# Gated scan, token mixer and two MLPs in one kernel: state sums in groups of 32 columns, and a new order of VectorE's and ScalarE's work in the weave

## The reference, cut to what matters

```
x = attn(q, k, v, a_re, a_im)            # 4 batches, 8 heads, 768 steps, 48 channels a head
    # per step t: S = a[t] * S + k[t] v[t]^T ; y[t] = q[t] . Re(S)   (a complex, |a| capped at 0.999)
x = x as [batch, 768, 384]
u = x + (relu(x^T w_tok1) w_tok2)^T      # token mixer, 768 -> 256 -> 768
x2 = u + relu(u w_ch1) w_ch2             # channel MLP 1, 384 -> 1536 -> 384
xn = (x2 - mean) / sqrt(var + 1e-6) * g
out = x2 + relu(xn w2_ch1) w2_ch2        # channel MLP 2
```

## Time and profile before

| | |
|---|---|
| median of three executions | 917.45 us (915.28 to 918.37) |
| the profiled execution | 917.37 us |
| its span, first to last instruction | 915.6 us |
| TensorE busy | 846.4 us, 92% |
| VectorE busy | 475.3 us, 52% |
| ScalarE busy | 415.0 us, 45% |
| GpSimd busy | 26.1 us, 3% |
| mean granted TensorE clock | 0.983 |

### The profile page before, as it was taken

How to read it: one execution, slowest core, us unless ns; L and a number is a source line. 1 busy time by engine, 2 the same in 40 slices (tenths; PEclk the granted TensorE clock), 3 DMA queues, 4 the chain that set the end, 5 groups by cost and what they waited for, 6 DMA issues and landing times. The chain is left out here.

```text
span 915.6 us, 15179 instructions
## 1 busy us (share of the span) xinstructions
PE 846.4 (92%) x6280; PEld 822.7 (90%) x6280; DVE 475.3 (52%) x821; ACT 415.0 (45%) x767; POOL 26.1 (3%) x39
## 2 busy tenths in 40 slices
PE   0757888999999999999999999999999999999998
PEld 0546777999999999999999999999999999999997
DVE  5875568877757775676673454253223313322121
ACT  6766358777727767657663332232112211211111
POOL 1010000000000000000000000000000000000000
PEclk9977899999999999999999999999999999999999
DMA  9935964444524555516342610000001002000000
GB/s 369 178 64 89 240 167 77 81 78 118 101 68 78 103 96 142 105 25 128 65 88 36 232 53 1 1 1 1 26 26 53 27 1 78 1 27 27 1 26 26
DMA packets 46839, 71.07 MB, mean 78 GB/s; under 512 B 5040, under 2 KB 38064, under 8 KB 46256
## 3 DMA queue, kind: packets, MB, share of 16 engines
q1 hardware_dynamic: 46768, 70.09, 32.6%
HBM read 42.86 MB, written 8.26 MB: 56 GB/s over the span
## 5 line engine op out<-in xcount | busy, mean ns | idle before, releaser
L701 ACT ACTIVATE hidden<-bank 128x384 fp32r<-128x384 f32 x192 | 93.7, 488 | 325.1 <-PE bank L333 324.7
L1015 DVE SCALAR_TENSOR_TENSOR hidden<-bank,hidden 128x384 fp32r<-128x384 f32 x192 | 105.8, 551 | 258.3 <-ACT hidden L701 258.3
L331 PE MATMUL bank<-ch,hidden 128*128 128x384 f32 x576 | 192.7, 335 | 3.7 <-DVE x_u L1023 3.6
L333 PE MATMUL bank<-ch,hidden 128*128 128x384 f32 x576 | 192.8, 335 | 0.0
L332 PE MATMUL bank<-ch,hidden 128*128 128x384 f32 x576 | 192.4, 334 | 0.0
L331 PEld LDWEIGHTS bank<-ch,hidden 128*128 128x128 f32 x576 | 108.1, 188 | 4.9 <-issue 4.8
L332 PEld LDWEIGHTS bank<-ch,hidden 128*128 128x128 f32 x576 | 108.1, 188 | 0.0
L333 PEld LDWEIGHTS bank<-ch,hidden 128*128 128x128 f32 x576 | 108.1, 188 | 0.0
L331 PE MATMUL bank<-turned_x,ch 128*128 128x384 f32 x288 | 102.9, 357 | 1.7 <-DVE turned_x L1097 1.7
L332 PE MATMUL bank<-turned_x,ch 128*128 128x384 f32 x288 | 97.1, 337 | 0.0
L333 PE MATMUL bank<-turned_x,ch 128*128 128x384 f32 x288 | 97.0, 337 | 0.0
(11 more groups left out here) (168 smaller groups left out, 1468.6 us busy)
## 6 DMA issues: line engine op xcount, KB each, us to landing
rows<-hats SPq DMA_DIRECT2D x126, 128.5 KB, 4.7
a_t<-in_a_rows_dram SPq DMA_DIRECT2D x20, 384.0 KB, 5.5
qk_t<-in_qk_rows_dram SPq DMA_DIRECT2D x19, 384.0 KB, 5.7
v_t<-in_v_cols_dram SPq DMA_DIRECT2D x24, 192.0 KB, 5.5
plain_ch<-in_moe_w_ch_dram SPq DMA_DIRECT2D x6, 768.0 KB, 10.6
out_dram<-x_u SPq DMA_DIRECT2D x24, 192.0 KB, 2.0
x_kept_dram<-x_u SPq DMA_DIRECT2D x18, 192.0 KB, 3.8
x_u<-x_kept_dram SPq DMA_DIRECT2D x18, 192.0 KB, 3.1
```

Of the source, the lines that this page charges most:

```text
L331: nc.tensor.matmul(ps, lhs_h, rhs_h, start=first, stop=False, skip_group_check=True)
L333: return nc.tensor.matmul(ps, lhs_l, rhs_h, start=False, stop=final, skip_group_check=True)
L701: nc.scalar.activation(hid_h[:, m % NHID, :], hid_ps[m % 2][:, 0:HALF], ACT.Relu).then_inc(hidden_rounded, 1)
L1015: nc.vector.scalar_tensor_tensor(out=hid_l[:, m % NHID, :], in0=hid_ps[m % 2][:, 0:HALF], scalar=0.0, in1=hid_h[:, m % NHID, :].bitcast(F3 ...
```

## The change

Three edits, on three engines.

TensorE: `chunk_state` cuts the 96 columns of each head in three groups of 32, and each group writes its own 32 partitions of the bank. 160 products become 480.

VectorE, in the slots: `turn_scan(n+1)` goes ahead of `mask(n,0)` (but in slot 6); `turns_wrapped` keeps its place behind step 0; in slots j = 3 `add_u` goes from behind the second step's `rest_hidden` to a place between `turns_wrapped` and `mask(n,1)`; `row_stats` and the `rest_x` of the even tiles go behind `log_sums`, ahead of the fourth step.

ScalarE, in the slots: the `round_x` of slots j = 3 and j = 5 go behind `log_magnitude`, ahead of `keep_x`; in slot 6 `keep_khat(n,1)` goes ahead of the table load, `angle` and the sines.

```diff
+    GROUP = P // 4
@@ ScalarE, slot
                 step(0)
                 keep_khat(n, 0)
+                if n == NT:
+                    round_piece(act, 5)
+                    growth(n + 1 - PAIRS)
+                    keep_khat(n, 1)
+                    use_turns()
+                    angle(n + 1 - PAIRS)
+                    step(1)
+                    prepare(n + 1, round_turns, sines)
+                else:
+                    prepare(n + 1, round_turns)
+                    step(1)
+                    prepare(n + 1, sines)
+                    keep_khat(n, 1)
+                prepare(n + 1, decays)
+                step(2)
+                use_logs()
+                prepare(n + 2, square, inverse_of_re, log_magnitude)
                 if j == ST:
                     for i in range(0, ST, 2):
                         round_x(b * NT + i)
                 if j == NT - 1:
                     round_x(b * NT + j - 1)
-                if n == NT:
-                    round_piece(act, 5)
-                    growth(n + 1 - PAIRS)
-                    use_turns()
-                    angle(n + 1 - PAIRS)
-                    step(1)
-                    prepare(n + 1, round_turns)
-                else:
-                    prepare(n + 1, round_turns)
-                    step(1)
-                prepare(n + 1, sines)
-                keep_khat(n, 1)
-                prepare(n + 1, decays)
-                step(2)
-                use_logs()
-                prepare(n + 2, square, inverse_of_re, log_magnitude)
                 keep_x(n, slow)
@@ VectorE, slot
-                mask(n, 0)
                 if n == NT:
+                    mask(n, 0)
                     step(0)
                     rest_piece(dve, 5)
                     mask(n, 1)
                     prepare(n + 1, turn_scan, turns_wrapped)
                 else:
                     prepare(n + 1, turn_scan)
+                    mask(n, 0)
                     step(0)
+                    prepare(n + 1, turns_wrapped)
                     if j == ST:
-                        for i in range(0, ST, 2):
-                            rest_x(b * NT + i)
-                    if j == NT - 1:
-                        rest_x(b * NT + j - 1)
-                    prepare(n + 1, turns_wrapped)
+                        add_u(2 * (b - 1))
                     mask(n, 1)
                 step(1)
                 prepare(n + 1, grown_qk, turn_hats)
                 ...
                 prepare(n + 2, log_sums)
+                if j == ST:
+                    row_stats(2 * (b - 1))
+                    for i in range(0, ST, 2):
+                        rest_x(b * NT + i)
+                if j == NT - 1:
+                    rest_x(b * NT + j - 1)
                 step(3)
@@ VectorE, the steps of the weave
-                            if m - first == FT + 1:
-                                add_u(2 * b)
-                            if m - first == FT + 2:
-                                row_stats(2 * b)
@@ TensorE, chunk_state
-                    last = nc.tensor.matmul(m_ps[0:D2, h * D:(h + 1) * D], khat[:, h * D2:(h + 1) * D2], v_head(n, h), start=True, stop=True)
+                    for lo in range(0, D2, GROUP):
+                        last = nc.tensor.matmul(m_ps[lo:lo + GROUP, h * D:(h + 1) * D], khat[:, h * D2 + lo:h * D2 + lo + GROUP], v_head(n, h),
+                                                start=True, stop=True)
```

## The result

| | before | after |
|---|---|---|
| median, timed side by side | 917.08 us (4 runs) | 906.66 us (4 runs, 906.01 to 908.63) |
| ratio, 95% interval | | 0.9891 (0.9868 to 0.9914) |
| profiled execution | 917.37 us | 906.01 us |
| its span | 915.6 us | 904.2 us |
| mean granted TensorE clock | 0.983 | 0.980 |

The change is worth 1.1%, 10.4 us by the medians. In a second session, on another chip, the same kernel took 906.26 us (4 runs) against 915.08 (9 runs): 0.9901 (0.9885 to 0.9917), 8.8 us. In the changed kernel the lines have moved by one to six: `turn_k` is L1248, `scores` L1257, `outputs` L1275 and L1279, `chunk_state` L1290, `mask` L956, `rest_hidden` L1021, `add_u` L1029, `up` and `down` L332 to L334, `lay_rows` L472.

The account below looks back on a forecast made before the run. TensorE's own work was taken to bound the weave, with a hats-and-DMA loop nearly as long. Sums 3.85, `add_u` 5.4, `turn_scan` 1.1, less 0.4 and 0.6, make 9.35 us: 917.37 to 908.0, range 905.5 to 914.5.

Parts of the forecast that it names:

- The second loop: Tile start, second scores, mask, hats, then 7.7 to 8.8 us of DMAs: nearly as long as TensorE's own loop.
- State sums in groups of 32: TensorE's state sums: 45 ns a round of three groups, 0.72 us for 16 rounds, 0.50 us saved a tile.
- Plain slots: Slots 10, 14, 16, 22 save the full 0.50, 2.0 us; the other four only their slack, 1.2 us.
- `add_u`: Slots 9, 15, 21: ahead of the second mask it removes TensorE's wait; 1.8 us each, 5.4 together.
- `turn_scan`: Ahead of the first mask: hats about 0.55 us earlier in slots 12 and 18, 1.1 for both; plain slots 0.
- Slot 6: The wait for `keep_khat` goes, but the copy delays the angle, hats and start of tile 7: 0.4 us lost.
- Slots 11, 17, 23: `rest_x` ahead of the fourth `rest_hidden` exceeds its 0.4 us of cover: 0.2 us lost each, 0.6 together.
- The prologue: State sums before the weave: 0.5 us saved after tile 4, some 0.15 elsewhere.
- rival (1): State sums: pairs come no faster than 29 ns, 915.2 us, or 26 ns, 912.9 us; chance 0.20 for both.
- Rival (2): Late landings take half the gain of plain slots and `add_u`: 911 to 912 us; chance 0.12.
- Rival (3): State sums: the three groups run one after the other, each sum 0.9 us longer, 924.6 us; chance 0.08.
- Rival (4): State sums: weight loads alone set the step, 31 ns, 906.8 us; chance 0.05.

Follow-up runs that it names:

- the second version beyond the change: The changed kernel with `grown_qk` ahead of the second mask (but in slot 6), `keep_khat(6,1)` and the `rest_x` of slots 11, 17, 23 put back: 902.70 us, 0.9870.
- The first version beyond the change: The changed kernel with `grown_qk` moved ahead of the second mask in all slots but 6: 904.03 us, 0.9871 of before.
- the third: The second version beyond the change, with the second step's `rest_piece` in slots 6 and 7 moved behind the hats: 899.46 us, 0.9821 of before.

## Why the prediction was right, and where its terms were off

The forecast was 908.0 with a range of 905.5 to 914.5, the profiled execution took 906.01 and the median was 906.66. The likeliest case came out, by its own steps, and 2 us better. Those 2 us are luck: 1.9 us of the prologue's gain go with the clock (below). Without them the profiled executions differ by 9.5 us, against a sum of 9.35; and this sum is so close because a term that was 0.9 too small (`turn_scan`) met a loss of 0.7 in slot 7 that had been put at nothing.

**The second loop.** The prediction's main claim was that tile start, second mask, hats and landing form a loop nearly as long as TensorE's own. It holds: every start from tile 7 to tile 22, but for tiles 12 and 18, now comes 0.045 us after its landing, halving the DMAs' bytes brings the plain slots to 18.1, and so does an earlier hat. In the plain slots its waits are too short to be counted in the view of waits (0.6 us from 250 us on, at the starts of tiles 13 and 19): the reader finds them only as a distance, 18.13 to 18.40 where TensorE's own work is 18.1. The waits of `turn_k` between 160 and 500 us grew to 2.4, about 2.5 having been forecast, but not by the forecast's reason: 1.8 of them stand ahead of tile 8 (0.5 before), and the plain slots add none that the view counts.

**State sums in groups of 32.** Forecast 0.72 us from first to last start, 0.50 saved. Measured 0.675 and 0.57. A round of three groups takes 42 to 43 ns instead of 45. That is the size of the moving side as scaled from `scores`; no run varied the moving columns, so that it is what binds fits and is not shown. The rest is the two ends: 0.152 at the entry (0.15 forecast) and 0.136 at the exit (0.15). TensorE's own loop of 18.64 - 0.50 = 18.14 came out at 18.07.

**Plain slots.** Forecast 2.0 for slots 10, 14, 16 and 22, and 1.2 for 8, 13, 19 and 20. Measured 1.6 and 1.45 (of it 0.32 in slot 8). The sum is right and the split isn't. Slot 14 had a slack of 0.9 and saved only 0.26, since the DMAs of tile 15 landed 8.41 us after their hats instead of 7.87. Slot 20 had none and saved 0.38, since those of tile 21 took 8.36 instead of 8.76.

These shifts are not noise. Tile 15's landing comes 8.36 to 8.42 us after its hats in all seven executions with groups of 32, full DMAs and `grown_qk` where it was, and 7.87 and 7.80 in the two kernels with whole sums. The traces show something that goes with it: packets of 16 KB on the profile's queue for instructions, 49 of them before and 54 in the changed kernel, which has 640 matmuls more. The DMA view from the end of the hats on, for tile 15 before (316.40 to 322.40 us) and after (311.47 to 317.47):

```profile
q1 hardware_dynamic: 835, 0.78, 99.7%
```

```profile
q1 hardware_dynamic: 826, 0.77, 96.5%
q8 instruction: 1, 0.02, 1.8%
```

Of the 34 landings of tiles 7 to 23 in these two profiles, 12 have no such packet starting between 0.2 us before the end of the hats and 5 us after it; they come 7.68 to 7.87 us after the hats. The other 22 have one; 20 of them come 8.09 to 8.76 after, and only tile 23's two (7.67 and 7.79) don't. Tiles 8, 11, 15 and 22 have none before and one after, tiles 12 and 13 the reverse. No run moves such a packet by itself, so this is a coincidence in time that explains the numbers and not a cause shown. It means that a slack read from one slot's landing is good to half a us when the program's length or timing changes.

**`add_u`.** Forecast 1.8 each, 5.4; measured 1.72, 1.87 and 2.03, together 5.6. The steps stand too: `add_u` starts at 324.58, 4.65 us after the tile's start (4.65 forecast), the hats end 9.99 after it (10.1), the landing is 8.2 later (8.2), and the slot is 18.24 (18.3). The experiment that puts `add_u` back costs 1.4 a slot, so this part alone carries 4.2.

**`turn_scan`.** Forecast 1.1 in slots 12 and 18, nothing in plain slots. Measured 2.0 and nothing. This is the mis-sized term: the hats came sooner as worked out (the experiment gives back 0.64 and 0.72, 0.55 having been forecast), but in slot 12 the DMAs of tile 13, without an instruction packet beside them now, also landed 7.72 us after their hats instead of 8.25 (the groups alone, too, bring 0.5 us there), and the scan behind the first mask would have cost slots 9, 15 and 21 another 1.0, a cover that the prediction counted into `add_u`.

**Slot 6.** Forecast 0.4 lost; measured 0.58, and 0.59 by the experiment. The wait for `keep_khat` went and tile 7 came no earlier, as said. What is not in the prediction is the wait of 2.0 for `rest_hidden`; it stands ahead of the same landing and costs nothing more.

**Slots 11, 17, 23.** Forecast 0.2 each; measured 0.21 and 0.24, and undone by the experiment.

**What the sum left out.** The prologue was given 0.65 and saved 2.5: 0.55 from tile 0 to tile 1 (0.29 of it lost again by tile 2), 1.36 from tile 4 to tile 5 and 1.09 from tile 5 to tile 6. The 0.57 of a state sum is in the first and the second of these; the forecast had only the second. The rest of the second, 0.8, and all of the third go with the clock: a stretch at 1.2 GHz ended sooner in slot 4, and one of 3.4 us from 133.6 us on didn't occur. The outputs of tile 4 and the entry to its sum take 3.0 us before, mostly at 1.2 GHz, and 2.0 after. The 1.09 is not the change's doing: two of the versions beyond it, which hold the whole change, have that stretch again and take 24.6 us from tile 5 to tile 6, as before the change; all kernels without it take 23.4 to 23.5. Whether the rest of the prologue's clock moves with the change is open, as the two profiled executions of the changed kernel differ there from each other. Against it slot 7 lost 0.74: tile 8's DMAs landed 8.49 us after their hats instead of 7.76. This one does go with the groups: 7.71 to 7.76 in the two kernels with whole sums, 8.01 to 8.64 in the ten with groups of 32 and full DMAs. The prediction gave slot 7 nothing.

**The chances.** Two thirds of the 0.20 for rival (1) are 0.13 and not 0.12, and its rest is 0.07 and not 0.10. Neither moves the forecast or its range.

**The rivals.** The feed (1) is refuted: 14.4 ns a pair, half of the 29 that any row of before shows. The Trainium skill, TensorE: Matmul & The Clock Gate, in its section on the 56 ns gap, states a floor of about 25 ns between the starts of back-to-back matmuls; by it the 48 pairs would be an estimated 1.2 us, and the trace has 0.675, so for groups of columns this floor doesn't hold, and the measurement decides. Rival (2), landings that take half of the gain, is true in kind and small in size: 1.7 us between tiles 9 and 23, by the half-size DMAs. Rival (3), groups one after the other, didn't come; its relative did in the run with 64 and 32 columns. Rival (4), weight loads alone at 31 ns a round, is refuted by the 42 to 43.

## What to carry to other kernels

Cut a narrow product into column groups of equal width, the same width through the whole run of instructions: three groups of 32 overlapped down to a round of 42 to 43 ns here, but each change of width costs 0.14 to 0.15 us. When a wait of the bounding engine goes, look for the loop behind it, here hats and layout DMAs, whose slack shows in no busy share and, once used up, hardly in the view of waits: compare the distance between like starts with the engine's own work. And put operations whose inputs are ready into idle time ahead of a waiting one, since what the landing's producer gains is gained at the end, as far as the landing is late (here 0.1 to 0.3 us a plain slot out of 1 us), while a removed wait ahead of a later wait is worth nothing. And compare the landings themselves before and after: the same DMAs took half a us more or less where an instruction packet fell among them.

## What the runs showed of the hardware that was not expected

- Pairs of a weight load and a matmul in three column groups of 32 start 14.4 ns apart on average, 48 in 0.675 us.
- Neighbouring products of 64 and 32 columns start 136 to 151 ns apart at each change of width, 3.4 us for 32 pairs.
- With the same program, TensorE was granted 1.2 GHz for 6.8 us behind its 3.4 us of idle time at tile 7 in one profiled execution and 2.4 GHz in another. It is worth 2.5 us in slot 7. Of the kernels here, those with the groups alone, the orders alone, `keep_khat` back, `rest_x` back, the half-size DMAs, the late scan, the columns cut as 64 and 32 and the second version beyond the change had it; before and the one with the late `add_u` didn't. The first version beyond the change, with 3.4 us of idle time, and the third, with 1.74, both had 3.4 us at 1.2 GHz there. What decides it is open.
- Halving the bytes of six layout DMAs made their last landing only 0.4 us sooner on average, 7.7 us after the hats instead of 8.1.
- The six layout DMAs land 7.7 to 7.9 us after the hats when no 16 KB packet of the instruction queue starts in the first 5 us of that time, and 8.1 to 8.8 when one does, but for the last tile (34 landings of two profiles; a coincidence in time, with no experiment on it).
